# A five-operation router normalisation step with a later cross-partition sum, two expert sums joined over six units, and activation splits placed two to a unit

## The reference

```python
def reference(q, k, v, w_gate, w1, w2, w_in, w_out):
    x = attention(q, k, v)                       # 4 batches x 8 heads, 576 tokens, masked
    x = x.reshape(2304, 512)
    # first network: 8 experts, all tokens through every expert
    logits = x @ w_gate
    P = np.exp(logits - logits.max())
    for _ in range(8):
        P /= P.sum(1, keepdims=True) + 1e-09
        P /= P.sum(0, keepdims=True) + 1e-09
        P *= N / E
    y = sum(P[:, e:e+1] * (np.maximum(x @ w1[e], 0.0) @ w2[e]) for e in range(8))
    # second network
    h = y @ w_in
    g = np.where(h > 0.0, h, np.exp(np.minimum(h, 0.0)) - 1.0)
    return g @ w_out                             # (2304, 512), float32
```

## Time and profile before

| | before |
|---|---|
| median of 3 timed runs | 2138.15 us (2137.84 to 2145.97) |
| time of the profiled execution | 2146.04 us |
| its span, first to last instruction | 2144.3 us |
| mean granted TensorE clock | 0.983 |
| busy share: TensorE matmul, VectorE, GpSimd, ScalarE | 96%, 69%, 49%, 43% |

### The profile page before, as it was taken

The page is one execution under the profiler, slowest core; times in us unless marked ns, Lnnn a source line. Parts: engine busy times, 40 slices in busy tenths (PEclk is TensorE's granted clock), DMA queues, the critical chain, the costliest instruction groups (busy, mean ns, idle before and its releaser), DMA issues.

```text
span 2144.3 us, 29144 instructions
## 1 busy us (share of the span) xinstructions
PE 2060.5 (96%) x10611; PEld 1842.8 (86%) x10611; DVE 1486.8 (69%) x2478; ACT 930.3 (43%) x1702; POOL 1050.5 (49%) x797
## 2 busy tenths in 40 slices
PE   5889998999999999999999999999999999999999
PEld 4878887998998889999899888898999899888888
DVE  3665887666666666666666778766666666678887
ACT  5883332333333433333333476533333333376675
POOL 2354543545454465454545546465454545546442
PEclk9988998999999999999999999999999999999999
DMA  7441111212122122221222211222221222211211
GB/s 142 94 81 40 59 59 41 78 59 79 59 71 68 59 71 68 63 76 60 79 59 72 66 60 59 89 74 65 67 71 60 79 60 74 65 60 60 89 60 58
DMA packets 159549, 147.64 MB, mean 69 GB/s; under 512 B 64688, under 2 KB 126384, under 8 KB 159408
## 3 DMA queue, kind: packets, MB, share of 16 engines
q1 hardware_dynamic: 159408, 145.79, 23.4%
HBM read 141.05 MB, written 4.72 MB: 68 GB/s over the span
## 4 chain that ended last, share of the span: by engine, by line
PE 81%; DVE 10%; ACT 5%; issue 3%; SPq 2%; DMA 0%; POOL 0%; DVEq 0%
PE psum L689 13%; PE psum L688 13%; PE psum L687 13%; PE psum L628 13%; PE psum L631 12%; PE psum L630 12%; DVE acc L1067 1%; DVE x_lo_a L986 1%; PE psum L562 1%; PE psum L586 1%; DVE prob L1083 1%; DVE w_lo L991 1%; DVE row_sum L1078 1%; PE psum L603 1%; SPq L382 1%
## 5 line engine op out<-in xcount | busy, mean ns | idle before, releaser
L480 POOL TENSOR_TENSOR w_lo<-w_raw,w_hi 128x1024 fp32r<-128x1024 f32 x120 | 294.4, 2453 | 934.0 <-ACT w_hi L816 934.0
L1067 DVE SCALAR_TENSOR_TENSOR acc<-psum,prob,acc 128x512 f32<-128x512 f32 x516 | 387.2, 751 | 291.9 <-PE psum L689 286.2
L689 PE MATMUL psum<-w_hi,h_lo 128*128 128x512 f32 x1440 | 570.5, 396 | 0.0
L688 PE MATMUL psum<-w_lo,h_hi 128*128 128x512 f32 x1440 | 568.7, 395 | 0.0
L687 PE MATMUL psum<-w_hi,h_hi 128*128 128x512 f32 x1440 | 566.8, 394 | 0.6 <-issue 0.6
L628 PE MATMUL psum<-x_hi_a,w_hi 128*128 128x384 f32 x1296 | 443.3, 342 | 22.7 <-DVE c L1024 20.7
L631 PE MATMUL psum<-x_hi_a,w_lo 128*128 128x384 f32 x1296 | 440.1, 340 | 0.0
L630 PE MATMUL psum<-x_lo_a,w_hi 128*128 128x384 f32 x1296 | 438.8, 339 | 0.0
L689 PEld LDWEIGHTS psum<-w_hi,h_lo 128*128 128x128 f32 x1440 | 272.3, 189 | 59.7
L687 PEld LDWEIGHTS psum<-w_hi,h_hi 128*128 128x128 f32 x1440 | 273.4, 190 | 47.8 <-issue 0.9
L688 PEld LDWEIGHTS psum<-w_lo,h_hi 128*128 128x128 f32 x1440 | 272.6, 189 | 47.9
(11 more groups left out here) (115 smaller groups left out, 2838.7 us busy)
## 6 DMA issues: line engine op xcount, KB each, us to landing
w_raw<-in_moe_w_dram SPq DMA_DIRECT2D x192, 512.0 KB, 3.6
w_raw<-in_moe_w_in_dram SPq DMA_DIRECT2D x24, 512.0 KB, 3.4
w_raw<-in_moe_w_out_dram SPq DMA_DIRECT2D x24, 512.0 KB, 3.7
v_l<-in_v_dram SPq DMA_DIRECT2D x24, 128.0 KB, 3.7
out_dram<-acc SPq DMA_DIRECT2D x2, 1536.0 KB, 6.1
raw_l_q<-in_q_dram SPq DMA_DIRECT2D x16, 144.0 KB, 3.4
raw_l_k<-in_k_dram SPq DMA_DIRECT2D x16, 144.0 KB, 4.0
raw_s_q<-in_q_dram SPq DMA_DIRECT2D x16, 144.0 KB
```

What stands on the lines that cost most here:

```text
L480: pool.tensor_tensor(w2_lo[n % 2][:, :, :], w2_raw[:, :, :], w2_hi[n % 2][:, :, :].bitcast(f32), ALU.subtract).then_inc(w2_lo_s, 1)
L688: pe.matmul(dst, h_hi[:, i, kk, js], w2_lo[s][:, i, :], start=False, stop=False)
L689: mm = pe.matmul(dst, h_lo[:, i, kk, js], w2_hi[s][:, i, :], start=False, stop=(i == 1))
L1067: ins = dve.scalar_tensor_tensor(a, y, 1.0 if bare else gate_of(n, j), a, ALU.mult, ALU.add)
```

## The change

- A router step has six VectorE operations instead of eight. `prob` becomes a part of a larger tile `prob_eps` with one more column (1e-9) and one more row (1e-9 / 128), which GpSimd sets once, so that both sums contain the epsilon and the two additions go.
- `sum_columns(u)` moves from before P2 to behind P4, and `sink_cols` from before `evict(u, 4)` to the end of VectorE's list for the unit.
- `rescale` goes. In u = 8 ScalarE multiplies the six tiles of `acc[0]` by their gate, between `snap` and the weights' high parts; VectorE's `evict(8, j)` waits for it. The tiles of `acc[1]` are added by VectorE's `join(j)`, one in each of the units 9 to 14.
- The low parts of x and of the ELU hidden layer are written as `scalar_tensor_tensor` (times 1.0, minus) instead of `tensor_tensor`.
- Blocks 0, 1, 2 of x are split in units 4, 5, 6 of a phase; blocks 3 and 4 in its last unit and 5 and 6 in the next first one, where the second of a pair comes behind `make_c21`. GpSimd's fourth combination is made one unit earlier.
- `turn_back` makes two tiles a unit in three units, one after `down(u, 0)` and one after `down(u, 2)`.
- In ELU units `make_u2` stands ahead of `split_w1_a`, as it already does in the others.

```diff
+        SINK_ALL = 5 * SINKHORN_STEPS
+        prob_eps = sb("prob_eps", [P, TT + 1, E + 1], f32)
+        prob = prob_eps[:, 0:TT, 0:E]
...
+        def x_splits(n):
+            p, m = PHASE[n], n - FIRST[PHASE[n]]
+            if n == LAST[p] and p + 1 < len(PHASES):
+                return [(p + 1, 3), (p + 1, 4)]
+            if m == 0 and p > 0:
+                return [(p, 5), (p, 6)]
+            if m in (4, 5, 6) and p + 1 < len(PHASES):
+                return [(p + 1, m - 4)]
+            return []
...
-                return {3: (1,), 4: (2, 3), 6: (4,)}.get(n - FIRST[p], ())
+                return {3: (1,), 4: (2, 3), 5: (4,)}.get(n - FIRST[p], ())
...
+            pool.memset(prob_eps[:, 0:TT, E:E + 1], EPS).then_inc(eps_made, 1)
+            pool.memset(prob_eps[:, TT:TT + 1, :], EPS / P).then_inc(eps_made, 1)
...
                 for j in range(HT):
                     down(u, j)
-                    if j < len(js_y):
-                        turn_back(p_y, js_y[j])
-                if u < SINKHORN_STEPS:
-                    sum_columns(u)
+                    if js_y and j in (0, HT - 1):
+                        turn_back(p_y, js_y[min(j, 1)])
                 if more:
                     p2(n)
                     p7(n)
                 down(u, HT)
                 if more:
                     p4(n)
+                if u < SINKHORN_STEPS:
+                    sum_columns(u)
                 down(u, HT + 1)
...
+                if u == U_BARE:
+                    act.wait_ge(sink_step, SINK_ALL)
+                    for j in range(GT):
+                        act.wait_ge(evicted, GT * (U_BARE - 1) + j + 1)
+                        act.activation(acc[0][:, j, :], acc[0][:, j, :], ACT.Copy,
+                                       scale=prob_eps[:, group_of(0) * GT + j, 0:1]).then_inc(rescaled, 1)
...
-                dve.tensor_tensor(lo, x_raw(p, o), hi.bitcast(f32), ALU.subtract).then_inc(x_lo, 1)
+                dve.scalar_tensor_tensor(lo, x_raw(p, o), 1.0, hi.bitcast(f32), ALU.mult, ALU.subtract)\
+                    .then_inc(x_lo, 1)
...
-            def rescale(j):
-                a, a1 = acc[0][:, j, :], acc[1][:, j, :]
-                dve.tensor_scalar(a, a, gate_of(FIRST[0], j), None, ALU.mult).then_inc(rescaled, 1)
-                dve.wait_ge(rescaled, 2 * j + 1)
-                dve.scalar_tensor_tensor(a, a1, gate_of(U_E, j), a, ALU.mult, ALU.add).then_inc(rescaled, 1)
+            def join(j):
+                a = acc[0][:, j, :]
+                dve.wait_ge(evicted, GT * (U_BARE + 1 + j) + j + 1)
+                dve.scalar_tensor_tensor(a, acc[1][:, j, :], gate_of(U_E, j), a, ALU.mult, ALU.add)\
+                    .then_inc(joined, 1)
...
                 if n == U_BARE:
-                    dve.wait_ge(rescaled, 2 * j + 2)
+                    dve.wait_ge(rescaled, j + 1)
...
-                dve.tensor_scalar(row_sum[:, :], row_sum[:, :], EPS, None, ALU.add).then_inc(sink_step, 1)
...
-                dve.tensor_scalar(col_inv[:, :], bank(AUX)[:, 0:E], EPS, None, ALU.add).then_inc(sink_step, 1)
...
-                if n + 1 < U and u >= 0 and is_elu(u):
+                if more:
+                    make_u2(n)
+                if n + 1 < U:
                     split_w1_a(n + 1)
                 if u >= 0 and is_elu(u):
                     elu_sum(u, E12, c12[u % 2][:, :], c12[u % 2][:, :])
                     evict(u, 0)
                     elu_lo(u, H12, c12[u % 2][:, :])
-                if more:
-                    make_u2(n)
...
                 if u >= 0:
                     evict(u, 5)
+                if U_BARE < u <= U_BARE + GT:
+                    join(u - U_BARE - 1)
                 if more and is_elu(n):
                     elu_lo(n, H21, c21[:, :])
+                if sink is not None:
+                    sink_cols(sink)
```

More of the change, by code:

```diff
@@ L219, in build @@
         ones_made = sem("ones_made")
+        eps_made = sem("eps_made")
         top_row = sem("top_row")
@@ L249, in build @@
         rescaled = sem("rescaled")
+        joined = sem("joined")
         evicted = sem("evicted")
@@ L302, in early_t @@
             if p + 1 < len(PHASES):
-                return {3: (1,), 4: (2, 3), 6: (4,)}.get(n - FIRST[p], ())
+                return {3: (1,), 4: (2, 3), 5: (4,)}.get(n - FIRST[p], ())
             return ()
[L306 to L313, removed]
         def y_tiles(u):
             for p, (net, _) in enumerate(PHASES):
[L318 to L321, removed]
+                m = u - LAST[p] - 1
+                if net == 0 and 0 <= m < GT // 2:
+                    return p, (2 * m, 2 * m + 1)
             return None, ()
@@ L860, in elu_hi, with y_copy @@
                 act.activation(h_blk(hblk), src, ACT.Copy).then_inc(h_hi_s, 1)
+            def y_copy(p, j):
+                act.wait_ge(y_t, y_count(p, j) + 1)
+                t0 = PHASES[p][1] * GTOK + j * P
+                act.activation(xT[:, :, t0:t0 + P], bank(AUX).rearrange("p (c n) -> p c n", c=DC), ACT.Copy)\
+                    .then_inc(y_copied, 1)
             act.wait_ge(pads_made, 2)
@@ L905, in _ @@
                     act.wait_ge(top_ready, 1)
-                    act.activation(prob[:, :, :], logits[:, :, :], ACT.Exp, bias=top_neg[:, :]).then_inc(prob_made, 1)
+                    act.activation(prob, logits[:, :, :], ACT.Exp, bias=top_neg[:, :]).then_inc(prob_made, 1)
+                p_y, js_y = y_tiles(u)
+                for j in js_y[:1]:
+                    y_copy(p_y, j)
                 if n < U:
-                    if (o := early_x(n)) is not None:
-                        split_x(PHASE[n] + 1, o)
-                    for x in late_x(n):
+                    for x in x_splits(n):
                         split_x(*x)
[L912 to L917, removed]
+                for j in js_y[1:]:
+                    y_copy(p_y, j)
                 if n < U and not is_elu(n):
@@ L1012, in elu_lo @@
                 dve.wait_ge(h_hi_s, 4 * n + b)
-                dve.tensor_tensor(lo, src, hi.bitcast(f32), ALU.subtract).then_inc(h_lo_s, 1)
+                dve.scalar_tensor_tensor(lo, src, 1.0, hi.bitcast(f32), ALU.mult, ALU.subtract).then_inc(h_lo_s, 1)
             def make_u2(n):
@@ L1041, in gate_of @@
                 e = (n - FIRST[PHASE[n]]) // U_E
-                return prob[:, group_of(n) * GT + j, e:e + 1]
-            def rescale(j):
-                a, a1 = acc[0][:, j, :], acc[1][:, j, :]
-                dve.tensor_scalar(a, a, gate_of(FIRST[0], j), None, ALU.mult).then_inc(rescaled, 1)
-                dve.wait_ge(rescaled, 2 * j + 1)
-                dve.scalar_tensor_tensor(a, a1, gate_of(U_E, j), a, ALU.mult, ALU.add).then_inc(rescaled, 1)
+                return prob_eps[:, group_of(n) * GT + j, e:e + 1]
+            def join(j):
[3 more added lines that the diff above has]
+                    .then_inc(joined, 1)
             def evict(n, j):
@@ L1060, in evict @@
                 if n == U_BARE:
-                    dve.wait_ge(rescaled, 2 * j + 2)
+                    dve.wait_ge(rescaled, j + 1)
+                if j == n - U_BARE - 2:
+                    dve.wait_ge(joined, j + 1)
+                if fresh and p == 1 and j == 0:
+                    dve.wait_ge(joined, GT)
                 if fresh and bare:
@@ L1129, in _ @@
                     elu_lo(u, H12, c12[u % 2][:, :])
-                if more:
-                    make_u2(n)
-                if n + 1 < U and not (u >= 0 and is_elu(u)):
-                    split_w1_a(n + 1)
-                if u == U_BARE:
-                    dve.wait_ge(sink_step, SINK_OPS * SINKHORN_STEPS)
-                    for j in range(HT):
-                        rescale(j)
                 if u == -1:
@@ L1152, in _ @@
                     evict(u, 2)
-                if u == U_BARE:
-                    for j in range(HT, GT):
-                        rescale(j)
                 if more:
-                    if (o := early_x(n)) is not None:
-                        split_x(PHASE[n] + 1, o)
-                    for x in late_x(n):
+                    for x in x_splits(n)[:1]:
                         split_x(*x)
@@ L1172, in _ @@
                     make_c21(n)
+                    for x in x_splits(n)[1:]:
+                        split_x(*x)
                     if is_elu(n):
                         elu_sum(n, E22, c22[:, :], c22[:, :])
-                if sink is not None:
-                    sink_cols(sink)
                 if u >= 0:
```

27 lines of the change are left out of this document (10 added, 17 removed).

## The result

| | before | after |
|---|---|---|
| median | 2142.06 us (4 runs, 2137.84 to 2148.82) | 2080.76 us (4 runs, 2078.51 to 2085.98) |
| ratio | | 0.9714, 95% interval 0.9677 to 0.9751 |
| profiled execution, span | 2146.04, 2144.3 us | 2078.70, 2076.9 us |
| granted clock, mean | 0.983 | 0.997 |

A fourth run of the kernel before, 2148.82 us, lifts its median from the 2138.15 us of three runs to 2142.06. The kernel became 2.9% faster. The forecast was 2094 with a range down to 2081: the direction was right, and so were the mechanisms of the three large terms, but the size was too small by 13 us.

What follows compares the result with a forecast made beforehand. TensorE was taken to set the pace, so only excesses over ordinary units could be won: 20.8 + 11.5 + 15.3 + 1.4 = 49.0 us. From 2146.04 this gives 2097; 2094 was taken, range 2081 to 2110 (forecast itself 2086 to 2102).

Steps and rivals of the forecast that it cites:

- router units: Eight units with a router step: 18.50 us becomes 15.90 each without the wait for the column sums, saving 20.8 us.
- rescale, unit 8: Unit 8, 27.40 us: scaling moves from VectorE to ScalarE and joins, saving 11.5 us, between 10.8 and 11.8.
- last units of phases: Last unit of each phase has one split of x instead of three ahead of U3: 15.3 us saved, 12 to 16.
- ELU units: ELU phases: units 1 to 3 gain 3.6 us, unit 4 loses 1.1, twice; net 1.4, between -4 and +6.
- low parts as another instruction: Low parts of x and the ELU hidden layer: the new form stands behind GpSimd too, so nothing is gained.
- ordinary units: Units without an excess: 15.60 us each in the first phase, TensorE never idle; no saving priced.
- rival (a): In router steps the multiply still stands behind both GpSimd instructions and P4 waits, some 10 us: 2107 us; chance 0.12.
- Rival (c): The splits' waits move to other units and cost 1.5 us at each of five phase changes: 2101 us; chance 0.12.
- rival (b): New form of the low parts is free of GpSimd; waits go in some ten ELU units: 2084 us; chance 0.10.
- what is taken as the start: Profiled execution, 2146.04 us, gives 2097; the timed median, 2138.15, ends at 2097 or 2089; 2094 was taken.

Runs made afterwards that it cites:

- padded kernel: Kernel before with an unused 128-byte-a-partition tile behind `prob`, no instruction changed, against the kernel before: 2132.5 us, ratio 0.9971.

## Why the prediction was wrong

By stages behind unit 1, the two first profiles differ by 1948.5 - 1890.5 = 58.0 us. The terms:

| term | forecast | measured |
|---|---|---|
| router units | 20.8 | 21.7 |
| rescale, unit 8 | 11.5 | 11.8 |
| last units of phases | 15.3 | 16.0 |
| ELU units | 1.4 | 3.7 |
| low parts as another instruction | 0 | 0 |
| ordinary units | not priced | 4.8 |
| sum | 49.0 | 58.0 |

- **Router: right.** The multiply ends at L480's end as forecast; rival (a) fell. But the prediction credits both halves of the edit, and the experiments give all to the dropped operations. I had worked out that `col_part` would be ready at 220.65, ahead of TensorE at 221.11, without drawing the conclusion that the sum need not move.
- **Rescale and splits: right**, each within 0.7 us. The six activations took 3.78 us against 3.7. Rival (c) fell in the first network; in ELU phases unit 4 did rise, from 16.5 us in an execution without the extra wait to 18.2, more than the 1.1 that was priced.
- **ELU units: mis-sized**, 1.4 against 3.7. 2.1 of this lies in phases 2 and 4, and 0.7 of that is the extra wait of the one profile before; against the padded kernel these phases gained 1.3 together, which is what was forecast, but by luck: in each of them units 1 to 3 gained 2.7 us instead of 1.8, since TensorE no longer waits around the transposes, and units 0, 4 and 6 lost about 2.1 instead of 1.1. The other 1.6 lies in phase 5, which the net left out, and there U2's new place alone brought it.
- **Low parts: right**, rival (b) at 0.10 fell.
- **Ordinary units: the step that failed.** The prediction took 15.60 us for every unit without an excess as a constant of the kernel, and so put these units at nothing without a reason. The padded kernel shows that 128 bytes of displacement make them shorter: from 327.54 to 326.66 us for the 21 units behind unit 8, from 469.2 to 466.4 for units 73 to 102, and 4.8 us over all of them. Nothing in the profile before shows that.
- **The sum.** With the terms as measured, 9.0 us more than forecast, the same working would have ended at 2085 instead of 2094. The last 4 us hang on what is taken as the start, and here the prediction guessed. It asked whether the timed runs below the profiled execution owe it to fewer losses of clock in the stretches that go, or to something else. The traces show both: the first stage differs by some 9.5 us whatever the kernel, and the stretches that go, mostly by their losses of clock, by some 5.7. Which of the two the median run had, no trace shows. From the three-run median the measured terms lead to 2138.15 - 58.0 = 2080.2, from the four-run median to 2142.06 - 58.0 = 2084.1; that the first is so near the measured 2080.76 is luck.

For the same reason the 58.0 us are those of one pair of executions. Against the padded kernel, which lost less clock, the change is worth 1938.0 - 1890.5 = 47.5 us behind unit 1, and 52.3 with the 4.8 of the tiles' place.

The separate ratios multiply to 0.9853 x 0.9943 x 0.994 x 0.9994 = 0.973, where the whole change has 0.9714. The 0.2% between them is the size of the ELU order and the turn-backs, but each ratio is uncertain by 0.3 to 0.4%, so the windows and not the ratios show that the parts add up.

## What to carry to other kernels

When a tiny VectorE operation takes two microseconds, look at what GpSimd runs beside it before moving who waits for it: one two-input operation that came early enough slipped in between two GpSimd instructions, and with the one ahead of it dropped, the later sum brought nothing more. A gain has to be taken from a baseline in the same condition as the profile: compare first the stages that the change does not touch. A tile that grows moves all tiles behind it, so test that with an unused filler before a small gain or loss is put down to the instructions.

## What the hardware showed that I had not expected

- The same matmuls at full clock and with TensorE never idle took 469.19, 466.40 and 468.20 us for 30 units with the later tiles 0, 128 and 160 bytes further; at 384 bytes it was 466.40 again.
- The same wait can cost clock or not. Of the eight router units before, each with a wait of TensorE of 1.6 us, four took about 19.3 us with clock lost and four 17.7. With the sum moved alone, none of the five waits of 1.0 us was followed by a loss, and two of the three of 2.0 us were. The waits left in the ELU phases after, the longest 1.6 us, cost none (1.00).
- A waiting VectorE operation with two SBUF inputs was let in at the end of the first of two back-to-back GpSimd instructions in all eight router steps after.
